# A fused delta-rule attention and two-layer MLP kernel: beta spread by TensorE, fillers and DVE work of the first pair placed elsewhere, gram products of the tiles a unit later

## The reference, cut to what matters

```python
# attention: batch 4, heads 8, sequence 768, head width 48; state is 48x48 per head
k_n = k / (norm(k) + 1e-6)
for t in range(S):
    y[:, :, t] = einsum('bhd,bhde->bhe', q[:, :, t], state)
    v_old = einsum('bhde,bhd->bhe', state, k_n[:, :, t])
    state = state + beta[t] * outer(k_n[:, :, t], v[t] - v_old)
x = y.transpose(0, 2, 1, 3).reshape(3072, 384)
x = ((x @ w_a) * (x @ w_b)) @ w_out          # 384 -> 1536 -> 384
h = x @ w_in                                 # 384 -> 2048
out = (maximum(h, 0) + alpha * minimum(h, 0)) @ w_out2   # 2048 -> 384
```

## Time and profile before

| | |
|---|---|
| median of the runs | 1062.45 us |
| the profiled execution | 1064.98 us |
| its span, first to last instruction | 1063.2 us |
| TensorE busy | 1028.3 us, 97% |
| VectorE busy | 574.1 us, 54% |
| ScalarE busy | 406.0 us, 38% |
| GpSimd busy | 107.1 us, 10% |
| mean granted TensorE clock | 0.982 |

### The profile page before, as it was taken

How to read it: one execution, slowest core, us unless ns; L and a number is a source line. 1 busy time by engine, 2 the same in 40 slices (tenths; PEclk the granted TensorE clock), 3 DMA queues, 4 the chain that set the end, 5 groups by cost and what they waited for, 6 DMA issues and landing times.

```text
span 1063.2 us, 23941 instructions
## 1 busy us (share of the span) xinstructions
PE 1028.3 (97%) x10055; PEld 855.4 (80%) x10055; DVE 574.1 (54%) x884; ACT 406.0 (38%) x776; POOL 107.1 (10%) x99
## 2 busy tenths in 40 slices
PE   7588999999999999999999999999999999999998
PEld 4445887888887889787889788789888788888898
DVE  4956975455496445476545468544458633322433
ACT  3524444555412434332435331434441333321443
POOL 1013673443000001000001000001000000000000
PEclk8689999999999999999999999999999999999999
DMA  8705999779695457496457597556556445766652
GB/s 139 141 17 156 295 310 301 237 235 320 170 258 181 149 148 251 139 253 198 158 157 221 164 238 217 157 165 204 183 164 192 151 148 166 238 194 194 190 184 84
DMA packets 195786, 203.80 MB, mean 192 GB/s; under 512 B 113696, under 2 KB 143408, under 8 KB 195680
## 3 DMA queue, kind: packets, MB, share of 16 engines
q1 hardware_dynamic: 192288, 201.52, 63.8%
q10 hardware_dynamic: 3264, 0.61, 0.3%
q0 software_dynamic: 128, 0.14, 0.1%
HBM read 166.04 MB, written 31.46 MB: 186 GB/s over the span
## 4 chain that ended last, share of the span: by engine, by line
PE 91%; ACT 4%; DVE 2%; issue 1%; DMA 1%; ACTq 1%; SPq 0%; DVEq 0%
PE bank L459 27%; PE bank L461 25%; PE bank L460 25%; PE bank L541 2%; PE bank L549 1%; PE bank L488 1%; PE bank L638 1%; PE bank L560 1%; PE bank L585 1%; PE bank L588 1%; PE bank L604 1%; PE bank L591 1%; ACT kz L755 1%; PE bank L632 1%; PE bank L635 1%
## 5 line engine op out<-in xcount | busy, mean ns | idle before, releaser
L854 ACT CAST g_hi<-g_sb 128x512 fp32r<-128x512 f32 x168 | 104.4, 621 | 258.5 <-DVE g_sb L1106 163.4
L1111 DVE SCALAR_TENSOR_TENSOR g_sb<-f_sb,neg_alpha,e_sb 128x512 f32<-128x512 f32 x96 | 78.3, 816 | 192.7 <-ACT f_sb L851 191.6
L459 PE MATMUL bank<-x_hi,w_two 128*128 128x512 f32 x432 | 171.3, 397 | 1.2 <-DVE x_lo L1095 1.2
L460 PE MATMUL bank<-x_lo,w_two 128*128 128x512 f32 x432 | 168.6, 390 | 0.0
L461 PE MATMUL bank<-x_hi,w_two 128*128 128x512 f32 x432 | 168.5, 390 | 0.0
L1117 DVE TENSOR_TENSOR g_lo<-g_sb,g_hi 128x512 fp32r<-128x512 f32 x168 | 121.7, 725 | 65.4 <-ACT g_hi L854 65.1
L459 PE MATMUL bank<-w_two,g_hi 128*128 128x384 f32 x384 | 133.3, 347 | 0.6 <-DVE g_lo L1117 0.6
L461 PE MATMUL bank<-w_two,g_lo 128*128 128x384 f32 x384 | 129.0, 336 | 0.0
L460 PE MATMUL bank<-w_two,g_hi 128*128 128x384 f32 x384 | 128.8, 335 | 0.0
L1106 DVE TENSOR_TENSOR g_sb<-e_sb,bank 128x512 f32<-128x512 f32 x72 | 49.4, 686 | 143.5 <-PE bank L461 143.2
L461 PE MATMUL bank<-m_hi,w_two 128*128 128x512 f32 x288 | 114.0, 396 | 0.0
(11 more groups left out here) (138 smaller groups left out, 1542.3 us busy)
## 6 DMA issues: line engine op xcount, KB each, us to landing
w_two<-split_scratch SPq DMA_DIRECT2D x340, 384.0 KB, 3.5
split_scratch<-w_two SPq DMA_DIRECT2D x68, 384.0 KB, 4.2
w_ring<-in_moe_w_out_dram SPq DMA_DIRECT2D x28, 192.0 KB, 4.0
k_tok<-in_k_dram SPq DMA_DIRECT2D x24, 192.0 KB, 4.9
q_tok<-in_q_dram SPq DMA_DIRECT2D x24, 192.0 KB, 5.1
out_dram<-o_sb SPq DMA_DIRECT2D x24, 192.0 KB, 3.5
w_ring<-in_moe_w_in_dram SPq DMA_DIRECT2D x16, 192.0 KB, 3.5
x_raw<-y_sb SPq DMA_DIRECT2D x30, 96.0 KB, 2.4
```

Source lines behind the costliest of these rows:

```text
L459: pe.matmul(dst, lhs_hi, rhs_hi, start=start, stop=False)
L460: pe.matmul(dst, lhs_hi, rhs_lo, start=False, stop=False)
L854: act.copy(g_hi[:, j % GR], g_sb[:, j % GR]).then_inc(gh_ok, 1)
L1111: dve.scalar_tensor_tensor(g_sb[:, j % GR], f_sb[:, f % 2], neg_alpha[:, f:f + 1], e_sb[:, f % 2], ALU.mult, ALU.add).then_inc(g_ok, 1)
```

## The change

Seven edits, all of order but the first two:

1. Beta is loaded by two DMAs instead of six, and ahead of the six for `k_raw` on ScalarE's queue. The rows of the second half of the heads have another token order; this was done by the DMAs, and is now done by TensorE: step `B` has 12 + 48 small products instead of 12 transposes. `B` comes first of all on TensorE, with 6 fillers behind it where 12 were, and 3 fillers instead of 1 between the first two `TRK`.
2. A new step `GC`: ScalarE copies the k·q products of chunk 1, second half, from PSUM to `kz0`; the mask of chunk 1 (`PT 1`) then works on `kz0` in place.
3. Fillers behind the last four `TR` of pair 1 (2 each) and behind each of its four `GG` (6 each). The fillers that wait for `solve` start at row 27 instead of 23 (16 instead of 24).
4. `PT 0` stands ahead of `H2`, `SQ 2` ahead of the rows, `KS 2` behind `H2`, `PT 1` behind `H1` of chunk 1, `GM` behind its `H4`. The 3 fillers between `HS` and `HY` of chunk 0 are gone.
5. `DG` and `PM` of pair 1 go into tile 0, and its solver starts 3 units later.
6. In the tiles from pair 2: `TR` at units 0, 1, 2, 4 (were 0, 1, 3, 5), `GG` at 3, 5, 7, 9 (were 2, 4, 6, 8), `DG` and solver one unit later.
7. The dependent stages stand at units 31, 33, ... instead of 30, 32, ...

```diff
-        seq += [("LV", 0), ("LV", 1)] + [("F", 0)] * 12 + flat(norms(0))
-        seq += [("TRK", 0)] + [("F", 0)] + [("TRK", 1), ("B",)] + [("F", 0)] * 3 + [("GK", 0, 0), ("GK", 1, 0)]
+        seq += [("LV", 0), ("LV", 1), ("B",)] + [("F", 0)] * 6 + flat(norms(0))
+        seq += [("TRK", 0)] + [("F", 0)] * 3 + [("TRK", 1)] + [("F", 0)] * 3 + [("GK", 0, 0), ("GK", 1, 0)]
...
-        seq += [("TRQ", b) for b in range(B)] + [("GQ", 0), ("GQ", 1)]
-        seq += [("TR", 1, g) for g in TR_ORDER] + [("GG", c, g) for g in range(2) for c in (2, 3)]
+        seq += [("TRQ", b) for b in range(B)] + [("GQ", 0), ("GQ", 1), ("GC",)]
+        for g in TR_ORDER:
+            seq += [("TR", 1, g)] + [("F", 0)] * (2 * (g >= 4))
+        for g in range(2):
+            for c in (2, 3):
+                seq += [("GG", c, g)] + [("F", 0)] * 6
+        seq += [("SQ", 2)]
         for n in range(1, ROWS + 1):
-            seq += [("ROW", 0, n)] + [("F", n)] * (2 * (n > R16 + 4))
+            seq += [("ROW", 0, n)] + [("F", n)] * (2 * (n > R16 + 8))
         seq += [("XT", 0)] + [("F", ROWS)] * 6
...
-                at[(0, 1, 3, 5)[n // 2]].append(("TR", p, g))
+                at[(0, 1, 2, 4)[n // 2]].append(("TR", p, g))
...
-                m = 30 + 2 * n
+                m = 31 + 2 * n
...
                 elif kind == "B":
-                    pe.wait_ge(beta_ld, 16 * NT)
+                    pe.wait_ge(beta_ld, 32)
                     for c in range(C):
-                        pe.transpose(bk[:, c * U:(c + 1) * U], beta_rows[:, c, :], ident[0:U, 0:U])
+                        pe.matmul(bk[:, c * U:c * U + UH], beta_rows[:, c, :], ident[0:U, 0:UH], start=True, stop=True)
+                    for c in range(C):
+                        for i in range(4):
+                            pe.matmul(bk[quad(3 - i), c * U + UH:c * U + U], beta_rows[:, c, quad(i)], ident[0:U, UH:U],
+                                      start=True, stop=True)
...
+                        pe.wait_ge(gc_ok, 1)          # in HY of chunks 0 and 1
...
+                elif kind == "GC":
+                    act.wait_ge(gq_full, 2)
+                    src = g0_bank[3][:, :].rearrange("p (w t) -> p w t", t=T)
+                    for h in range(2):
+                        ins = act.copy(kz0[tok(1, h), :, 1, 1 + h], src[tok(1, h)])
+                    ins.then_inc(gc_ok, 1)
```

More of the change, by code:

```diff
@@ L138, in build @@
         gk_full, gk_free, gq_full, pt0_ok = sem("gk_full"), sem("gk_free"), sem("gq_full"), sem("pt0_ok")
-        gm_ok, pm_ok = sem("gm_ok"), sem("pm_ok")
+        gm_ok, pm_ok, gc_ok = sem("gm_ok"), sem("pm_ok"), sem("gc_ok")
         dg_ok, dgv_ok, solve = sem("dg_ok"), sem("dgv_ok"), sem("solve")
@@ L239, in build @@
-        for kind in ("H2", "H3", "H4", "HS", "HY"):
-            seq += [(kind, 0)] + [("F", 0)] * 3 + beside0.get((0, kind), [])
-        for kind in ("H1", "H2", "H3", "H4", "HY", "HS"):
-            seq += [(kind, 1)] + [("F", 0)] * 3 + beside0.get((1, kind), [])
+        seq += [("PT", 0, 0), ("PT", 0, 1)]
+        beside0 = {(0, "H2"): [("KS", 2), ("SQ", 3)], (0, "H4"): [("KS", 3), ("KN", 1)], (0, "HS"): [("KI", 1), ("LV", 2)],
+                   (0, "HY"): [("XL", 0, 0, T)], (1, "H1"): [("PT", 1, 0), ("PT", 1, 1), ("WS", 0)], (1, "H2"): [("WS", 1)],
+                   (1, "H3"): [("WS", 2)], (1, "H4"): [("GM", 2), ("GM", 3), ("WS", 3), ("WT", 0), ("WT", 1)]}
@@ L243, in build @@
+        for c, kinds in enumerate((("H2", "H3", "H4", "HS", "HY"), ("H1", "H2", "H3", "H4", "HY", "HS"))):
+            for kind in kinds:
+                seq += [(kind, c)] + [("F", 0)] * (3 * ((c, kind) != (0, "HS"))) + beside0.get((c, kind), [])
         seq += [("XL", 0, T, P), ("LV", 3), ("WT", 2)] + [("F", 0)] * 16 + [("XS", 0, kc) for kc in range(KC)]
-        seq += [("DG", 3, 0), ("DG", 3, 1)]
         def tile_units(i):
@@ L266, in beside @@
                 for n, g in enumerate(TR_ORDER):
-                    at[(0, 1, 3, 5)[n // 2]].append(("TR", p, g))
+                    at[(0, 1, 2, 4)[n // 2]].append(("TR", p, g))
                 for g in range(2):
-                    at[2 + 4 * g].append(("GG", 2 * p, g))
-                    at[4 + 4 * g].append(("GG", 2 * p + 1, g))
-                for j in range(2):
-                    at[8 + j].append(("DG", 2 * p, j))
-                    at[10 + j].append(("DG", 2 * p + 1, j))
-            s = 12 if p > 1 else 1
+                    at[3 + 4 * g].append(("GG", 2 * p, g))
+                    at[5 + 4 * g].append(("GG", 2 * p + 1, g))
+            else:
+                at[29] += [("PM", 2), ("PM", 3)]
+            for j in range(2):
+                at[(9 if p > 1 else 0) + j].append(("DG", 2 * p, j))
+                at[(11 if p > 1 else 2) + j].append(("DG", 2 * p + 1, j))
+            s = 13 if p > 1 else 4
             at[s].append(("IN", p))
@@ L711, in _ @@
         def _(act):
+            for h in range(2):
+                act.dma_start(beta_rows[:, :, HALVES[h]], beta.rearrange("b (u two) (c t) -> two (b u) c t", two=2, t=T)[h]
+                              ).then_inc(beta_ld, 16)
             load_k(act, 0, 1)
-            for rows, w, h, t in token_parts():
-                act.dma_start(beta_rows[w, :, rows],
-                              beta.rearrange("b (u two) (c t) -> two (b u) c t", two=2, t=T)[h][w, :, t]).then_inc(beta_ld, 16)
             act.wait_ge(vinit, 2)
@@ L1045, in _ @@
                     else:
+                        if c:
+                            dve.wait_ge(gc_ok, 1)
                         for h in range(2):
                             t = tok(1, h)
-                            ins = dve.tensor_tensor(kz0[t, :, c, 1 + h], src[t],
+                            ins = dve.tensor_tensor(kz0[t, :, c, 1 + h], kz0[t, :, c, 1 + h] if c else src[t],
                                                     upper[t, 1].unsqueeze(1).to_broadcast([T, UH, T]), ALU.mult)
```

4 lines of the change are left out of this document (removed).

## The result

The changed kernel took 1053.96 us, the median of five runs (1053.85 to 1057.86); the kernel before, measured with it on the same chip, 1063.56 us (1062.26 to 1064.95). The ratio is 0.9924, 95% interval 0.9902 to 0.9947: 9.6 us faster, where 13.7 us were forecast (from 1062.45 to 1048.8). The time lies in the predicted range, in its upper half. The profiled execution took 1053.85 us, its span is 1052.1 us, 11.1 less than before. The two profiles show 1.5 us more than the medians: that of before took 1.4 us more than the median of its kernel, that of after is the fastest of its five runs.

The account below looks back on a forecast made before the run. Bound: TensorE's own list up to 64.38 us, then the chain of small stages up to the first tile. Terms -1.9 - 6.1 - 4.0 - 1.7 = -13.7 us, from 1062.45 to 1048.8 us; range 1045 to 1056.

Parts of the forecast that it names:

- The start: Up to pair 1's gram stage: pair 0's gram products start at 13.4 instead of 15.27 us, -1.9 (+1.1 to -3).
- the price of `B`: Beta's step at the start: its 60 small products take 4 us, between bounds of 1.7 and 6.9.
- the upper bound of 6.9: At the start: `B`'s products at 0.115 us each; pair 0's gram products would then start 1.1 us later than before.
- This leaves room for hardly more than 3: At the start: pair 1's four q loads, landing at 31.2 us, leave room for 1.9 us and hardly more than 3.
- rival B: At the start: beta lands late, at 12.4 us, and `B` takes its upper 6.9; -3.4 in all, 1059.1 us; chance 0.07.
- Gram stage and fillers: Pair 1's gram stage up to `H2`: steps at full clock, then 28 fillers, 15.7 instead of 21.8 us, -6.1.
- Rival A: In the gram stage: the clock stays at half, +5.8 there, -1.8 in all, 1060.6 us; chance 0.07.
- Short stages: Before the first tile: mask and norm gone behind `H4` (-1.7), `HY` at once behind `HS` (-2.3), together -4.0 us.
- Tiles: The four tiles preparing pairs 2 to 5: the gram step's wait of 0.86 us is halved, -1.7 us (0 to 3.5).
- The stall: In those four tiles: the 0.86 us wait for ScalarE's copy moves to the transposes, where 0.43 remains.
- Hidden, with 1.8 us left: First tile, ahead of unit 30: `PM` and `XT` take 6.2 us of VectorE, delaying TensorE nowhere, with 1.8 us to spare.
- Rival D: In the tiles: all 32 gram steps and transpose pairs wait 0.86 us at shared banks; +12.0, 1074.5 us; chance 0.05.

Follow-up runs that it names:

- e1: The changed kernel with the 12 wide products of `B` made as transposes again; 1056.28 us, ratio 0.9933.
- e8: The changed kernel with beta's load, step and place as before, and 12 instead of 28 fillers behind the last gram step; 1051.13 us, ratio 0.9872.
- e10: As e8, with pair 0's twelve loads of v moved behind pair 1's loads of k and q on SP's queue; 1053.88 us, ratio 0.9901.
- e11: As e1, with pair 0's v loads moved behind pair 1's k and q, and 12 fillers behind the last gram step; 1046.88 us, ratio 0.984.
- e7: The kernel before with only the filler edit (part 3 of the change); 1058.86 us, ratio 0.9951.
- e4: The changed kernel without the 8 fillers among pair 1's transposes and the 24 behind its four gram steps; 1056.17 us, ratio 0.9932.
- e2: The changed kernel with beta's load, step and place as before; 1052.30 us, ratio 0.9892.
- e3: The changed kernel with the placements in the tiles from pair 2 on as before (parts 6 and 7 undone); 1059.91 us, ratio 0.9961.

## Why the prediction was right, and where not

**The start (-1.9 forecast, -0.6 measured).** The step that failed is the price of `B`: 4 us taken, 6.6 measured (4.59 to 11.17), near the upper bound of 6.9. The split was wrong the other way round: "12 of the products are as wide as the old ones (0.12 us)" took a transpose's row for a product's; they cost 0.44, and the 48 small ones 0.03. Both kernels ran this at half the clock: the five fillers recorded right behind `B` took 2.34 us in each, where five took 1.24 in the gram stage at clock 1.00. The gram products of pair 0 then came 2.6 us later than before, which the prediction had at that bound as 1.1. That this cost nothing at the next stage, and that e1, with 4.5 us of it taken back, gained nothing there, shows the second mistake. "This leaves room for hardly more than 3" saw the queue of loads as a remote bound; it was the bound, and it lies in the place of v's loads ahead of pair 1's q. With the old beta and the old order of loads the stage starts at 42.4 us (e8), with the loads alone moved at 41.4 (e10), with the cheap early `B` alone at 42.1 (e1); only e11 takes away both, and the stage starts at 38.9, 3.1 us earlier than in the changed kernel. Of rival B the first half came true (a dear `B`), not the late beta.

**Gram stage and fillers (-6.1 forecast, -5.8 measured).** Right in mechanism and size. Steps of 2.95 us at clock 1.00, 27 to 28 fillers in 6.22 us; e7 gives the same 16.07 us alone, and e4, which takes the fillers out, brings the half clock back at the place where the earlier trace rows had it. Rival A is refuted. The rule that stands beside it, which the Trainium skill has in "TensorE: Matmul & The Clock Gate", Part 4, that a transpose does not count as busy for the clock as other products do, fits e4, where the clock fell at 42.7 us behind transposes and rose again only among the fillers, at 56.4; but TensorE had also been idle there for 1.4 us, so e4 does not single it out. What the prediction left lying there is that the solver was done 2.5 us before `H2` (53.44 + 2.10 = 55.54), and 6.1 to 6.3 us of fillers still ran first; e8 collects 3 us of that.

**Short stages (-4.0 forecast, -1.7 measured).** The sum itself holds where no code is late: from `H2` to `H1` of chunk 1 e8 shows -3.98. Then it is 0.5 us longer to the first tile, and that was not in the sum. It lies in the last ten DMAs to `x_raw`: from the first issue to the last landing they take 4.5 us in the trace of before, 5.0 in the changed kernel's, e2's and e8's, and 4.9 in that of e7, which has the fillers alone. So it does not come with the moved work of VectorE; why they take longer is open. In the changed kernel `H2` to `H1` is 11.90 us instead of 10.06, and the 1.84 us between them are the two late waits, 0.80 + 1.04. This is the largest miss, and the step that failed is a term put at nothing. The prediction followed which engine waits for which, and the code itself was not among the things waited for.

**Tiles (-1.7 forecast, -3.1 measured).** The stall did move to the transposes, but 0.2 us of it and not 0.43; this brings 1.0 us more than forecast. Against it, "Hidden, with 1.8 us left", said of the masks and `XT` ahead of unit 30 of the first tile, failed. In the timelines of VectorE, GpSimd and TensorE after:

```profile
148.97 2.29 DVE L972 STREAM_TRANSPOSE xt<-inv 128x1024 f32<-128x1024 f32 x1
151.11 1.80 DVE L1015 TENSOR_TENSOR pt<-pt,upper 128x512 f32<-128x512 f32 x1
152.93 3.29 DVE L1018 TENSOR_TENSOR kz<-kz,upper 64x512 f32<-64x512 f32 x2
156.14 0.68 DVE L1015 TENSOR_TENSOR pt<-pt,upper 128x512 f32<-128x512 f32 x1
156.83 1.39 DVE L1018 TENSOR_TENSOR kz<-kz,upper 64x512 f32<-64x512 f32 x2
158.14 0.67 DVE L1126 TENSOR_TENSOR g_sb<-e_sb,bank 128x512 f32<-128x512 f32 x1
```
```profile
150.89 1.48 POOL L1181 TENSOR_TENSOR v_raw<-v_raw,knorm 128x768 f32<-128x768 f32 x1
152.32 1.46 POOL L1191 TENSOR_TENSOR w_two<-w_ring,w_two 128x384 fp32r<-128x384 f32 x1
153.74 1.93 POOL L1181 TENSOR_TENSOR v_raw<-v_raw,knorm 128x768 f32<-128x768 f32 x1
```
```profile
158.87 0.50 PE L465 MATMUL bank<-x_hi,w_two 128*128 128x512 f32 x1 [1.21 <-DVE g_sb L1126]
```

`XT` and the four rows of masks took 9.3 us (148.97 to 158.22) where 6.2 were priced, mainly since the first two rows took 5.1 us and the same two again 2.1. The 3.1 us too much used up the 1.8 that were left, and TensorE waited 1.21 us. The slow rows stand beside GpSimd's work on v and the weights (150.89 to 155.67 us), the quick ones behind it, and so it is in the traces of e1 and e2; that GpSimd slows them was not tested by a run. Before, there was a wait of 0.6 us for `g_lo` late in that tile instead. e3, which keeps this part, has the same wait, and its tiles are 0.8 us longer than before. e3 undoes the other two parts and loses 3.9 us, 2.7 of them in waits; the 1.2 that stand in no wait are not explained. Rival D (waits at the banks) did not occur.

Of the 13.7 us the medians show 9.6 and the profiles 11.1. In the profiles 1.3 us are missing at the start, 0.3 in the gram stage and 2.3 in the short stages, and the tiles gave 1.4 more, so that terms that failed offset each other. Two reasons for what is missing are settled by the experiments: loads of v that stood ahead of pair 1's k and q (behind them the dear products of `B` were hidden), and code that arrives late. Why a packet of instructions starts late is open. It is not other traffic of this core: at 61.33 us in e10 and 63.77 in the changed kernel a block was entered, its packet started 3.2 and 2.6 us later, and the traces have no other DMA packet in between. Both follow a late one, so that one may delay the next. Its effect scatters: the changed kernel's profiles differ by 3.8 us at the first tile with the same program, and its runs lie between 1051.4 and 1057.9 us, e11's between 1046.6 and 1047.1.
